# A new order of the work ahead of block 0, and v of tile 3 weighed and q and k of tiles 4 and 5 split one step sooner

## The reference

```python
for t in range(S):
    m_new = max(f[t] + m, i[t]); f_stab = exp(f[t] + m - m_new); i_stab = exp(i[t] - m_new)
    C = f_stab * C + i_stab * outer(v[t], k[t]);  n = f_stab * n + i_stab * k[t]
    y[t] = sigmoid(o[t]) * (C @ q[t]) / max(abs(n . q[t]), 1)
x = relu(x @ w_in) ** 2 @ w_out          # first dense layer
x = elu(x @ w2_in) @ w2_out              # second dense layer
```

## Time and profile before

| | |
|---|---|
| median of 3 runs | 826.26 us (824.21 to 826.77) |
| the profiled execution | 827.41 us, its span 825.7 us |
| busy in the span | PE 99%, DVE 76%, ACT 60%, POOL 34% |
| block 0's first matmul | 36.33 us |
| first dense layer ends, second starts | about 426 us |

### The profile page before, as it was taken

The page is one execution under the profiler, slowest core; times in us unless marked ns, Lnnn a source line. Parts: engine busy times, 40 slices in busy tenths (PEclk is TensorE's granted clock), DMA queues, the critical chain, the costliest instruction groups (busy, mean ns, idle before and its releaser), DMA issues.

```text
span 825.7 us, 14869 instructions
## 1 busy us (share of the span) xinstructions
PE 818.5 (99%) x5251; PEld 813.6 (99%) x5251; DVE 625.1 (76%) x1466; ACT 493.9 (60%) x1096; POOL 280.5 (34%) x289
## 2 busy tenths in 40 slices
PE   9999999999999999999999999999999999999998
PEld 7899999999999999999999999999999999999998
DVE  5788698898897988987965786776777686867533
ACT  4789676776767767777648754444444444444433
POOL 2654332322222423211102354333434343333432
PEclk9989999999999999999999999999999999999999
DMA  7674544443653443436132300000000000000000
GB/s 241 226 234 139 163 116 108 107 124 93 156 152 86 138 107 107 110 104 156 32 106 71 106 2 5 27 4 27 4 27 4 26 4 25 5 27 4 21 6 25
DMA packets 23089, 66.58 MB, mean 81 GB/s; under 512 B 2886, under 2 KB 10214, under 8 KB 20454
## 3 DMA queue, kind: packets, MB, share of 16 engines
q1 hardware_dynamic: 22438, 64.18, 27.2%
q10 hardware_dynamic: 576, 1.44, 0.5%
HBM read 60.87 MB, written 4.03 MB: 79 GB/s over the span
## 4 chain that ended last, share of the span: by engine, by line
PE 95%; DMA 2%; DVE 1%; ACT 1%; issue 1%; POOL 0%; SPq 0%; DVEq 0%; POOLq 0%
PE hps L1030 43%; PE acc L1044 41%; PE att L954 5%; PE att L916 2%; PE att L945 2%; PE att L933 1%; DMA raw<-in_qk 1%; DVE gate L671 0%; PE acc L916 0%; DMA m_rows<-x 0%; POOL wout L421 0%; DMA x<-in_gates_ends 0%; PE att L959 0%; ACT win L540 0%; DVE x L726 0%
## 5 line engine op out<-in xcount | busy, mean ns | idle before, releaser
L1030 PE MATMUL hps<-xth,win 128*128 128x384 f32 x1280 | 350.2, 338 | 0.1
L1044 PE MATMUL acc<-wout,ghi 128*128 128x320 f32 x1536 | 345.5, 312 | 0.0
L1030 PE MATMUL hps<-xtl,win 128*128 128x384 f32 x768 | 259.4, 338 | 0.0
L1044 PEld LDWEIGHTS acc<-wout,ghi 128*128 128x128 f32 x1536 | 259.0, 189 | 0.0
L1044 PE MATMUL acc<-wout,glo 128*128 128x320 f32 x768 | 237.8, 310 | 0.0
L1030 PEld LDWEIGHTS hps<-xth,win 128*128 128x128 f32 x1280 | 230.8, 189 | 0.6 <-DVE xtl L734 0.5
L477 POOL TENSOR_TENSOR glo<-hact,ghi 128x384 fp32r<-128x384 f32 x128 | 134.4, 1050 | 210.1 <-ACT ghi L644 210.1
L1030 PEld LDWEIGHTS hps<-xtl,win 128*128 128x128 f32 x768 | 144.8, 189 | 0.0
L1044 PEld LDWEIGHTS acc<-wout,glo 128*128 128x128 f32 x768 | 144.5, 188 | 0.0
L641 ACT ACTIVATE hact<-hact 128x384 f32<-128x384 f32 x128 | 67.3, 526 | 116.8 <-DVE hact L884 116.8
L851 DVE TENSOR_TENSOR glo<-hact,ghi 128x384 fp32r<-128x384 f32 x128 | 75.6, 591 | 63.5 <-ACT hact L603 62.5
(11 more groups left out here) (146 smaller groups left out, 741.0 us busy)
## 6 DMA issues: line engine op xcount, KB each, us to landing
raw<-in_qk SPq DMA_DIRECT2D x20, 960.0 KB, 7.1
wts<-m_rows SPq DMA_DIRECT2D x24, 512.0 KB, 8.7
kvo<-in_kvo SPq DMA_DIRECT2D x21, 484.0 KB, 7.9
x<-in_w_all SPq DMA_DIRECT2D x12, 352.0 KB, 6.3
wts<-in_w_all SPq DMA_DIRECT2D x12, 352.0 KB, 3.0
q_of_three<-in_q_trios SPq DMA_DIRECT2D x20, 180.0 KB, 3.4
out_x<-hsum SPq DMA_DIRECT2D x16, 160.0 KB, 1.8
x<-in_w_all ACTq DMA_DIRECT2D x4, 352.0 KB, 6.0
```

What stands on the lines that cost most here:

```text
L1030: last = nc.tensor.matmul(hps[t % 2][:, 0:NT], win[:, j, w, :], x[:, kk, :], start=(i == 0), stop=(i == len(parts) - 1))
L1044: last = nc.tensor.matmul(acc[u][:, 0:DM], g[t % GR][:, cols], wout[:, j, w, :], start=(j == 0 and i == 0), stop=(j == NF - 1 and i == 2))
```

## The change

- `RING` weight slices (0 to 5) are loaded in one go by SP; 4 and 5 went out behind the loads of tile 3 before.
- ACT, ahead of block 0: out_gate(1) ahead of exponents(2); slices 0 to 3 ahead of x_hi(0), then slices 4 and 5, exponents(3, 0), x_hi(1), exponents(3, 1), first_state(0), x_hi(2), out_gate(3). first_state(1) moves into step 0.
- DVE: gate_recip(1) ahead of finish(0).
- PE: tile 1 is transposed into bank hps[1] instead of A0, so that tile 1 waits for no x_lo and tile 2 only for that of tile 0; tile 2's transposes stand ahead of the three of int_exp; state_added(1) moves behind first_product(0).
- POOL: make_wv(1) behind mask(3) and keep_last(3); make_wv(3) in step 2 instead of 3.
- The splits of q and k of tiles 4 and 5 stand one step sooner on ACT, DVE and POOL: `split_at` gives each its step. For tile 4, split_k_hi stands in step 2, split_q_hi and split_k_lo in step 3, split_q_lo in step 4. From tile 6 on nothing moves.

```diff
-FIRST_STATES = {2: 2, 4: 3}
+FIRST_STATES = {0: 1, 2: 2, 4: 3}
+def split_at(t, ahead):
+    for g in range(B, TILES):
+        if start_of(g) - ahead - (g < 2 * T) == t:
+            return g
+    return None
...
         def x_bank(g):
-            return A0 if g < T else A2
+            return (A0, hps[1], A0)[g] if g < T else A2
...
-            for n in range(4):
+            for n in range(RING):
                 load_w(sp, n)
             load_qk(3)
             load_kvo(3)
             load_m(3)
-            for n in range(4, RING):
-                load_w(sp, n)
...
                 if n == 4:
-                    make_wv(1)
                     mask(T)
                     keep_last(T)
+                    make_wv(1)
...
-                        if t == 3:
+                        if t == 2:
                             make_wv(T)
...
-                        g = tile_at(t, -1)
-                        if g is not None and g >= B:
+                        g = split_at(t, 1)
+                        if g is not None:
                             split_q_lo(g, 0)
                             split_q_lo(g, 1)
...
+            out_gate(1)
             exponents(2, 0)
             exponents(2, 1)
-            out_gate(1)
             out_gate(2)
-            for n in range(2):
+            for n in range(4):
                 split_hi(n)
                 split_out_hi(n)
-            x_hi(0, 0, 0, A0)
-            for n in range(2, 4):
-                split_hi(n)
-                split_out_hi(n)
-            x_hi(1, 0, 1, A0)
-            first_state(0)
-            exponents(3, 0)
-            x_hi(2, 0, 2, A0)
-            exponents(3, 1)
-            first_state(1)
+            x_hi(0, 0, 0, x_bank(0))
             for n in range(4, EARLY):
                 split_hi(n)
                 split_out_hi(n)
+            exponents(3, 0)
+            x_hi(1, 0, 1, x_bank(1))
+            exponents(3, 1)
+            first_state(0)
+            x_hi(2, 0, 2, x_bank(2))
             out_gate(3)
...
-                        g = tile_at(t, -3)
-                        if g is not None and g >= B:
+                        g = split_at(t, 3)
+                        if g is not None:
                             split_k_hi(g)
-                        g = tile_at(t, -2)
-                        if g is not None and g >= B:
+                        g = split_at(t, 2)
+                        if g is not None:
                             split_q_hi(g)
...
             weigh(1)
+            gate_recip(1)
             finish(0)
             weigh(2)
-            gate_recip(1)
             finish(1)
-            x_lo(0, 0, 0, A0)
+            x_lo(0, 0, 0, x_bank(0))
             gate_recip(2)
             finish(2)
...
-                        g = tile_at(t, -2)
-                        if g is not None and g >= B:
+                        g = split_at(t, 2)
+                        if g is not None:
                             split_k_lo(g)
...
                 if g == 0:
                     pe.wait_ge(s["p_ready"], 1)
-                elif g < T:
-                    pe.wait_ge(s["xt_ready"], g)
-                else:
+                elif g == 2:
+                    pe.wait_ge(s["xt_ready"], 1)
+                elif g >= T:
                     pe.wait_ge(s["state_ready"], to_state(g + 1))
...
             state_added(0)
+            x1_transposed(2)
             pe.wait_ge(s["int_exp"], 1)
...
-            x1_transposed(2)
-            state_added(1)
```

More of the change, by code:

```diff
@@ L814, in _ @@
             weigh(1)
+            gate_recip(1)
             finish(0)
             weigh(2)
-            gate_recip(1)
             finish(1)
-            x_lo(0, 0, 0, A0)
+            x_lo(0, 0, 0, x_bank(0))
             gate_recip(2)
             finish(2)
-            x_lo(1, 0, 1, A0)
-            x_lo(2, 0, 2, A0)
+            x_lo(1, 0, 1, x_bank(1))
+            x_lo(2, 0, 2, x_bank(2))
             dve.wait_ge(s["int_ps"], 1)
```

## The result

The changed kernel takes 830.52 us (median of 7; 828.74 to 830.83) beside 825.38 us for the kernel before in the same comparison (823.83 to 827.8). The ratio is 1.0058, 95% interval 1.0043 to 1.0073: it is slower, by some 4.8 us by the ratio (the two medians are 5.1 us apart), where 1.0 us was forecast. Its profiled execution took 830.83 us with a span of 829.1 us, against 825.7 us before.

A forecast was written before the change was run, and what follows sets the result against it. PE, busy 818.5 of 825.7 us, bounds the kernel. A gain of 0.3 us up to scores(3) and 1.3 us more idle in step 4 make 1.0 us later: 826.26 + 1.0 = 827.3 us, range 824.2 to 829.9.

The forecast's parts named there:

- What bounds it: Whole kernel: PE bounds it; at stake are waits of 1.1 and 1.4 us, 3.4 us of low clock, the slow start.
- Ahead of block 0: Start up to scores(3): first product at 34.9 us instead of 36.33, scores(3) end at 41.7 instead of 42.0.
- The bounds: Load of m of tile 3 behind slices 4 and 5: no cost, or 3.0 us, some 2.3 reaching x_hi(2).
- "paper" argument: First product: 1.4 us sooner only on paper, as state_added(1) now stands behind it; idle falls from about 1.2 to 0.9 us.
- Step 2, the wait: ACT's split_k_hi(4) waits for its load ahead of first_state(2): PE waits 2.7 us instead of 1.4, state_added(3) at 50.7 us.
- The figure for a transfer by itself: Load of q and k of tile 4, 960 KB: 4.3 us estimated by the skill's fit, against 7.5 and 7.1 us traced.
- Nothing there reaches PE: The other earlier splits of tiles 4 and 5, on DVE, POOL and ACT: none delays PE.
- The term at zero: Earlier splits of tile 5: no cost to PE, the load arriving near 64 us and ACT wanting it near 68.
- The clock: Behind the wait in step 4: the same 6.8 us at the low level, 3.4 us lost in both kernels.
- The second rival: Behind the wait in step 4: the low clock lasts longer, 829.0 us, or 830.7 if by twice that; chance 0.23.
- The sum: Whole kernel: 0.3 us gained up to scores(3), 1.3 us more idle in step 4, together 1.0 us later, 827.3 us.

The follow-up runs named there:

- tile 5 alone: The changed kernel, but of the earlier splits only those of tile 5 remain; 824.89 us, 1.0001 of the kernel before.

## Why the prediction was wrong

*What bounds it.* Right in its rows, wrong in one reading. The trace of before shows a fall of the clock behind the 1.4 us wait, and I took it as a property of the kernel. It was one of that execution, and of 12 of the 85 that came later (18 more with a shorter one).

*Ahead of block 0.* x1_transposed(2) at 32.63 us, forecast 32.6. The first product at 36.08, forecast 34.9: m of tile 3 landed 8.3 us after its issue, where I took the old 6.3 us and said that 7 us of distance to the loads ahead make them free. The bounds held it (no cost, or some 2.3 us at x_hi(2)), the choice was wrong by 1.2 us. The "paper" argument was right: the first product starts 0.25 us sooner than before, and yet scores(3) start 1.35 us later, since state_added(1) now lies behind it and part of that work ran at the low clock: the six matmuls of line 935 took 1.29 us at 38.15. In this execution the clock had risen at about 33 us and fell again at about 37, behind the wait of 1.86 us, to come back at 40; I had no fall here. I had scores(3) 0.3 us sooner. How much of this is the order and how much the execution is open: over all traces scores(3) start between 39.9 and 41.5 us with the old order and between 39.7 and 42.0 with the new one. In the runs this term is not the loss: the kernels with the same order and the old splits are at 0.9985 and 0.9989.

*Step 2, the wait.* Right in its mechanism and its size. ACT was to reach line 495 at 47.2 us after a start at 37.7; it started at 38.39 and reached it at 48.36. The load landed 7.1 us after its issue (forecast 7.1 to 7.5), PE's wait was 2.74 us (2.7), state_added(3) came 1.30 us later than scores(3) alone account for (1.3); that it came at 52.39 and not at 50.7 us is the start. Moving first_state ahead of it takes the wait away.

*The figure for a transfer by itself.* The 4.3 us estimated from the Trainium skill's page (DMA: Bandwidth & Descriptors, section "Anatomy of one DMA — SWDGE (gpsimd) path") was not borne out; the changed kernel's own row is 7.1 us, with other transfers in flight. The page's fit is for one transfer on the GpSimd path, and SP issues this one; no run here has it by itself.

*"Nothing there reaches PE".* Wrong for tile 5. I had costed split_k_lo and split_q_lo by their own durations and by who waits for them, and not what they do to work beside them. The term at zero was 0.0016, some 1.3 us. The intervals alone would let it be nothing; the traces show the wait, 0.5 us in the changed kernel and 1.0 us with tile 5 alone.

*The clock.* This is the step that failed: "so I count the same 6.8 us at the low level, 3.4 us lost in both kernels". By the means it falls in every execution of the changed kernel, in the kernel before as in its trace in 12 of 85 and for a shorter time in 18. So the 3.4 us stood in the profiled execution of before, but not in the median that I carried the difference to, and taking them as lost in both kernels put the clock's part of the change at nothing. The longer wait turns an occasional loss into a regular one. Filled with work, the changed kernel takes 2.8 us less. The second rival had the clock for a culprit, but through a longer stretch in the changed kernel, and that did not come: its trace has 6.8 us. A longer stretch is what the splits on the kernel before show (10.2 us).

The sum, then, from the kernel with the old split steps (0.9985) to the changed one (1.0058), 6.0 us: 2.7 us of wait, 2.8 us of clock (measured by filling), 1.3 us of tile 5; that makes 6.8, within the intervals of its terms. Against the kernel before, with its own 1.4 us of wait and an estimated 0.8 us of clock, 4.8 us are left. My 1.0 us was the growth of the wait (1.3) less a start that I had 0.3 us sooner, and nothing else.

## To carry to other kernels

When a wait of before is followed by a low clock, ask how often that happens before counting it in both kernels: the spread of the times and the mean clock of each execution tell, a single trace doesn't. Work that is moved forward in an in-order queue brings its own input's arrival with it; here a split that nobody wanted for another 10 us held back a small copy that PE needed at once, and any such split should stand behind it. And a prefetch moved ahead of another may, as here, only choose which of the two is late.

## What the runs showed of the hardware that was not expected

The same wait does not bring the same clock each time. With waits of 1.1 and 1.4 us it fell in the traced executions (for 3.4 and 6.8 us), but by their means not in ten of eleven and 55 of 85; with a wait of 2.7 us it fell in all seven, and 16 matmuls on zeros in the gap kept it up (granted 1.00 where it had been 0.50). Where between 1.4 and 2.7 us this turns was not measured. And a DVE operation of 0.29 us took 2.53 us beside POOL's split, a factor of nearly nine, for an operation that looked like cover.
